# Three blocks of 512 tokens instead of four of 384 in a fused attention, dense and two-expert kernel

## The chip, the cores and the metric

The kernel runs on one core of a Trainium2 chip. The metric is device time in microseconds of the whole program, from one launch. A core has TensorE (PE; PEld is its weight load), VectorE (DVE), ScalarE (ACT), GpSimd (POOL), SyncE (SP) and 16 DMA engines, which run side by side and meet at semaphores.

## The reference, cut to what matters

```python
# attention: 2 batches, 8 heads, 768 positions, head size 64; a window of 128 keys and 4 sinks
x = attention(q, k, v)                        # becomes 1536 tokens x 512
h = x @ w_in                                  # dense layer, 512 -> 2048
x = (h - tanh(h)) @ w_out                     # 2048 -> 512
noisy = x @ w_gate + log1p(exp(x @ w_noise)) * noise      # 8 experts
top2 = indices of the two largest of noisy;  w = softmax over these two
for e in range(8):                            # 512 -> 1024 -> 512
    out[chosen e] += w * (relu(x @ w1[e]) @ w2[e])
```

All of it is float32. The kernel splits each operand of a large product into a rounded part (hi) and the rest (lo) and multiplies three times: hi by hi, lo by hi, hi by lo.

## The kernel before

The order of the instructions on each engine is written out by hand; engines wait on semaphores that count up. There are three stages.

1. Attention, pair of heads by pair of heads. Its output goes through two PSUM banks into `xT_hi` and `xT_lo` (transposed tokens), 384 positions at a time.
2. The dense layer, block by block of `BLK` = 384 tokens (`KB` = 3 tiles of 128, `NBLK` = 4 blocks). For each of 16 chunks `fc` of the hidden axis, TensorE runs `hidden(blk, fc)` (12 matmuls, 4 chunks of the model axis by 3 products, into bank 0 or 1), ScalarE and VectorE make h - tanh(h) in place and split it (`block_hidden`), and two chunks later TensorE runs `project` (3 matmuls for each of the `KB` tiles, summed over `fc` in banks 2 to 4). Block 0 is written out; blocks 1 to 3 are a hardware loop. In the next block's first chunks lies the routing of the one before: `gate_turn`, `gate_route` and `gate_end` turn the block's output rows (`turn_tokens`, 4 transposes a tile) and multiply them by the gate weights (`route`, 4 products a tile, 8 records in the trace), then VectorE chooses two experts (`route_noise`, `route_choose`), `rank_tokens` counts, `route_place` gives each token a row, and GpSimd's `scatter` sends each tile's rows to `sorted_x` in two indirect DMAs, one for each choice.
3. The experts, as 31 tiles of 128 sorted tokens, in order of expert. A tile has `up` (24 matmuls) and `down` (24). Between them its hidden rows go to memory and back (`hid_out`, `hid_in`, both on ScalarE's queue), so that VectorE can transpose them in 32x32 blocks. Weights come in a ring of two experts; SyncE asks for an expert's four pieces in two halves each (L610), GpSimd splits each piece (L672, L674). The splits and the scatters share GpSimd's queue.

Around the change the order is this. Behind the last block TensorE runs `turn_rows(0)`, the routing steps without cover, `up(0)`, `rank_tokens`, `turn_rows(1)`, `turn_hidden(0)`, `up(1)`, `down(0)`, and `down(1)`, in which `turn_rows(2)` sits: that one needs rows which are loaded only behind the very last scatter (SyncE L594 to L595). SyncE then waits until the ring slot of the first expert is free and asks for the third expert's weights (L598 to L612).

At the end GpSimd gathers each token's two results from `sorted_y` (`gather`, 12 tiles twice, L750), scales and adds the first six tiles (`combine`, L762 and L765), while VectorE adds the last six (L1424), and SyncE writes them out. Before the gathers of a block GpSimd waits for a number of stored tiles (`stores_i`), worked out for that block:

```python
            for blk in range(NBLK):
                stores = pool.value_load(stores_i[0:1, blk, kk:kk + 1], min_val=16, max_val=16 * TILES)
                pool.wait_ge(scattered, 16 * TOP * TT)
                pool.wait_ge(ys_stored, stores)
                for i in range(blk * KB, blk * KB + KB):
                    gather(kk, rows, i)
                    if kk == 0 and i >= 2:
                        scale(i - 2)
                    if kk == 1 and 2 <= i < TT - LATE + 2:
                        combine(i - 2)
```

Of the kernel before, what the change touches and what calls it, by code (L numbers as in the profile page):

```python
# [39 lines left out]
def build(nc, q, k, v, w_in, w_out, w_gate, w_noise, noise, w1, w2, out, n_sink, window):  # L40
# [11 lines left out]
    TT = TOK // P  # L52
    BLK = S // 2
    KB = BLK // P
# [6 lines left out]
    HALF = FC // 2  # L61
    CAP = TOK
    QUAD = 4
    LANE = P // QUAD
    LATE = 2 * KB
    SCALE = float(D) ** -0.5
# [5 lines left out]
    W0 = n_sink  # L72
    assert 2 * D == P and H // 2 == CH and QT == 6 and KB == 3 and n_sink <= SK and window <= P

# [3 lines left out]
    with ExitStack() as ctx:  # L78
# [41 lines left out]


        X_HI = take(PAIRS * S)
        X_LO = take(PAIRS * S)
        xT_hi = place_at("xT_hi", X_HI, [2 * PAIRS, BLK], F32R)
        xT_lo = place_at("xT_lo", X_LO, [2 * PAIRS, BLK], F32R)
        gathered_a = place_at("gathered_a", X_HI, [TT, DM])
        y_rows_all = place_at("y_rows", X_LO, [KB, DM])
        y_rows = [y_rows_all[:, kk, :] for kk in range(KB)]
        assert KB * DM == CH * BLK

# [67 lines left out]
        rank_t = bank[7][:, P:P + KB * E].rearrange("p (i e) -> p i e", e=E)  # L198
        r_ln_t = bank[5][:, 0:KB * E].rearrange("p (i e) -> p i e", e=E)
        r_is_zero_t = route_table(E)  # L200
# [47 lines left out]
        part([2 * G * BLK])  # L248
        x2T = [part([DM]) for u in range(2)]

# [86 lines left out]

        ys = place_at("ys", X_LO + KB * DM, [DM])
        behind_rows = X_LO + (KB + 1) * DM
        xs = place_at("xs", behind_rows, [DM])  # L340
        hid = place_at("hid", behind_rows + DM, [FE])
        xsT_at = behind_rows + DM + FE
        xsT_hi = [place_at(f"xsT_hi{b}", xsT_at + 2 * b * DM, [DM], F32R) for b in range(2)]
        xsT_lo = [place_at(f"xsT_lo{b}", xsT_at + (2 * b + 1) * DM, [DM], F32R) for b in range(2)]
        assert xsT_at + 4 * DM <= X_LO + PAIRS * S

# [7 lines left out]
        part([FE])  # L354
        hidT_lo.append(place_at("hidT_lo_last", xsT_at + 2 * DM, [FE], F32R))
        assert FE == 2 * DM
# [136 lines left out]
        def _(sp):  # L493
# [295 lines left out]
        def _(act):  # L789
# [25 lines left out]
            def attn_out(p, half):  # L815
                act.wait_ge(attn_ready, 2 * p + half + 1)
                act.copy(xT_hi[:, half * PAIRS + p, :], attn_bank[half][:, 0:BLK]).then_inc(attn_act, 1)

# [206 lines left out]
        def _(dve):  # L1025
# [29 lines left out]
            def attn_out(p, half):  # L1055
                dve.wait_ge(attn_act, 2 * p + half + 1)
                at = half * PAIRS + p
                dve.tensor_tensor(xT_lo[:, at, :], attn_bank[half][:, 0:BLK], xT_hi[:, at, :].bitcast(F32),
                                  ALU.subtract).then_inc(attn_dve, 1)

# [43 lines left out]
            def block_rows(blk, scattered_blocks=None):  # L1104
                dve.wait_ge(y_ready, blk * KB + 2)
                if scattered_blocks is not None:
                    dve.wait_ge(scattered, 16 * TOP * KB * scattered_blocks)
                dve.tensor_copy(y_rows[1], bank[3][:, :]).then_inc(x2_dve, 1)

            def block_turned(blk, kk):  # L1110
                dve.wait_ge(x2_turned, blk * KB + kk + 1)
                dve.tensor_copy(x2T[0][:, :], bank[5][:, :]).then_inc(x2T_dve, 1)

# [86 lines left out]
            block_rows(0)  # L1200
            dve.wait_ge(route_loaded, 96)
            dve.wait_ge(consts_ready, 13)

            dve.sem_inc(ranks_read, 1)
            with dve.Fori(1, NBLK) as blk:

                for fc in range(FC):
                    block_hidden(blk, fc)
                    if fc < 2:
                        block_turned(blk - 1, 2 * fc)  # L1210
# [218 lines left out]
        def _(pe):  # L1429
# [73 lines left out]
            def hidden(blk, fc):  # L1503
# [68 lines left out]
            def turn_tokens(kk):  # L1572
                for c in range(CH):
                    last = pe.transpose(bank[5 + kk % 2][:, c * P:(c + 1) * P],  # L1574
                                        y_rows_all[:, kk, c * P:(c + 1) * P], ident[:, :])
                last.then_inc(x2_turned, 1)

            def route(kk):
                for c in range(CH):
                    last = pe.matmul(bank[7][:, kk * 2 * E:(kk + 1) * 2 * E],  # L1580
                                     x2T[kk % 2][:, c * P:(c + 1) * P], w_route[:, c, :],
                                     start=c == 0, stop=c == CH - 1)
# [36 lines left out]
            pe.wait_ge(attn_dve, 2 * PAIRS)  # L1619
            pe.wait_ge(route_loaded, 96)  # L1620
            with pe.Fori(1, NBLK) as blk:
                for fc in range(FC):
                    hidden(blk, fc)

                    if fc < 3:
                        (gate_turn, gate_route, gate_end)[fc](blk - 1)
                    if fc == 7:
# [71 lines left out]
            turn_rows(0)  # L1699
            for step in (gate_turn, gate_route, gate_end):  # L1700
                step(NBLK - 1)
# [59 lines left out]
```

## Time and profile before

| what | value |
|---|---|
| median of 3 runs | 734.25 us (729.37 to 735.9) |
| the profiled execution, its own time | 733.36 us |
| its span, first to last instruction | 731.4 us |
| TensorE busy | 717.3 us, 98% |
| GpSimd busy | 445.5 us, 61% |
| VectorE busy | 372.2 us, 51% |
| ScalarE busy | 225.8 us, 31% |
| mean granted clock of TensorE | 0.997 |

The profiled execution took 1.96 us more than its span; that is what lies around the instructions. Times of the trace count from the span's start. The end of a matmul is modelled, so the pace of matmuls is read from the starts of two of them, not from the duration of one.

### The profile page before, as it was taken

The page shows a single profiled execution, that of the slowest core. Times are in us where ns is not written, and L with a number is a line of the kernel's source. Part 1 is how long each engine was busy: PE and PEld are TensorE (multiplying, and loading weights), DVE is VectorE, ACT ScalarE, POOL GpSimd, SP SyncE. Part 2 cuts the span into 40 slices and gives each one's busy share as a digit, 9 for nine tenths or more (in the row PEclk, how much of TensorE's full clock was granted, in tenths as well). Part 3 has the DMA queues.
Part 4 walks back from the last instruction along what each step waited for, and adds up shares of the span by engine and source line. Part 5 has one row for each costly group of instructions (what it writes and reads, how often), then busy time and mean ns, then how long its engine had stood idle before and what let it go on. Part 6 is the DMA issues. An engine that isn't in the chain of part 4 may idle for free.

```text
span 731.4 us, 12987 instructions
## 1 busy us (share of the span) xinstructions
PE 717.3 (98%) x3792; PEld 608.7 (83%) x3793; DVE 372.2 (51%) x908; ACT 225.8 (31%) x530; POOL 445.5 (61%) x252
## 2 busy tenths in 40 slices
PE   7999999999999999999999989999999999999997
PEld 6677899999989999999987868888888888888886
DVE  4777532233523442344246556565656555665644
ACT  6999622223222422332222122121121121221212
POOL 6988998000300030003976996959995999986774
PEclk9999999999999999999999999999999999999999
DMA  8743385000100020004373478869785978758776
GB/s 273 283 147 97 111 302 229 0 1 1 73 14 1 0 86 0 0 0 156 117 297 120 125 225 284 262 210 302 244 271 178 323 240 293 269 169 265 224 234 218
DMA packets 69838, 121.46 MB, mean 166 GB/s; under 512 B 8240, under 2 KB 35504, under 8 KB 69296
## 3 DMA queue, kind: packets, MB, share of 16 engines
q1 hardware_dynamic: 28000, 63.92, 25.9%
q10 hardware_dynamic: 37968, 44.58, 17.8%
q0 software_dynamic: 3840, 12.59, 5.4%
q8 instruction: 16, 0.26, 0.2%
q14 instruction: 14, 0.11, 0.0%
HBM read 81.74 MB, written 39.32 MB: 166 GB/s over the span
## 4 chain that ended last, share of the span: by engine, by line
PE 90%; DMA 5%; SPq 2%; DVE 1%; POOL 1%; issue 1%; ACT 0%; ACTq 0%; POOLq 0%; DVEq 0%
PE bank L1689 20%; PE bank L1657 20%; PE bank L1514 18%; PE bank L1564 18%; PE bank L1467 4%; PE bank L1458 3%; PE bank L1440 2%; DMA hid_lanes<-hid_by_lane 2%; PE bank L1580 2%; DMA hid_by_lane<-hid 1%; SPq L524 1%; DMA arena<-in_k 1%; PE bank L1574 1%; POOL sorted_x L720 1%; DMA xs<-sorted_x 1%
## 5 line engine op out<-in xcount | busy, mean ns | idle before, releaser
L720 POOL DMA_INDIRECT sorted_x<-y_rows,arena x24 | 23.5, 980 | 210.7 <-DVEq L1178 204.6
L674 POOL TENSOR_TENSOR ring<-ring_raw,ring 128x2048 fp32r<-128x2048 f32 x32 | 147.6, 4613 | 2.5
L1689 PE MATMUL bank<-ring,hidT_hi 128*128 (+1 forms) x448 | 138.5, 390 | 3.7 <-DVE hidT_lo L1262 3.7
L1657 PE MATMUL bank<-ring,xsT_hi 128*128 (+1 forms) x496 | 134.0, 392 | 0.4 <-DVE xsT_lo L1225 0.4
L672 POOL TENSOR_TENSOR ring<-ring_raw,ones 128x2048 fp32r<-128x2048 f32 x32 | 115.3, 3602 | 27.0 <-DMA ring_raw<-in_moe_w 26.9
L1564 PE MATMUL bank<-w_out_sb,gated_hi 128*128 128x512 f32 x384 | 119.8, 393 | 0.0
L1657 PEld LDWEIGHTS bank<-ring,xsT_hi 128*128 128x128 f32 x496 | 93.4, 189 | 20.1 <-issue 0.8
L1689 PEld LDWEIGHTS bank<-ring,hidT_hi 128*128 128x128 f32 x448 | 83.8, 188 | 21.9 <-issue 4.7
L1097 DVE TENSOR_TENSOR bank<-bank,arena 128x384 f32<-128x384 f32 x64 | 36.2, 566 | 123.4 <-ACT arena L857 121.7
L1689 PE MATMUL bank<-ring,hidT_lo 128*128 (+1 forms) x224 | 87.2, 389 | 0.0
L1514 PE MATMUL bank<-xT_hi,w_in_hi 128*128 (+1 forms) x256 | 86.9, 340 | 0.0
L1514 PE MATMUL bank<-xT_hi,w_in_lo 128*128 (+1 forms) x256 | 86.3, 337 | 0.0
L1514 PE MATMUL bank<-xT_lo,w_in_hi 128*128 (+1 forms) x256 | 85.9, 336 | 0.0
L1564 PEld LDWEIGHTS bank<-w_out_sb,gated_hi 128*128 128x128 f32 x384 | 70.9, 188 | 12.2
L1657 PE MATMUL bank<-ring,xsT_lo 128*128 (+1 forms) x248 | 76.8, 391 | 0.0
L1564 PE MATMUL bank<-w_out_sb,gated_lo 128*128 128x512 f32 x192 | 75.8, 395 | 0.0
L857 ACT ACTIVATE arena<-bank 128x384 f32<-128x384 f32 x64 | 31.5, 492 | 140.9 <-PE bank L1514 133.2
L951 ACT CAST hidT_hi<-bank 128x512 fp32r<-128x512 f32 x56 | 30.4, 590 | 132.4 <-PE bank L1689 85.8
L1241 DVE STREAM_TRANSPOSE bank<-hid_lanes 128x512 f32<-128x512 f32 x56 | 62.0, 1153 | 18.3 <-DMA hid_lanes<-hid_by_lane 18.2
L1657 PEld LDWEIGHTS bank<-ring,xsT_lo 128*128 128x128 f32 x248 | 46.8, 189 | 9.9
L1101 DVE TENSOR_TENSOR gated_lo<-bank,gated_hi 128x384 fp32r<-128x384 f32 x64 | 35.7, 558 | 37.8 <-ACT gated_hi L862 37.8
L943 ACT ACTIVATE hid<-bank 128x512 f32<-128x512 f32 x31 | 18.6, 599 | 112.8 <-PE bank L1657 107.9
(205 smaller groups left out, 1060.9 us busy)
## 6 DMA issues: line engine op xcount, KB each, us to landing
ring_raw<-in_moe_w SPq DMA_DIRECT2D x48, 512.0 KB, 5.5
hid_by_lane<-hid ACTq DMA_DIRECT2D x28, 512.0 KB
hid_lanes<-hid_by_lane ACTq DMA_DIRECT2D x28, 512.0 KB
ring_raw<-in_moe_w SPq DMA_DIRECT2D x8, 1024.0 KB, 6.5
sorted_y<-ys ACTq DMA_DIRECT2D x31, 256.0 KB
xs<-sorted_x ACTq DMA_DIRECT2D x100, 64.0 KB
sorted_y<-zeros SPq DMA_DIRECT2D x1, 4864.0 KB, 25.7
arena<-in_k SPq DMA_DIRECT2D x8, 520.0 KB, 4.5
```

Source lines behind the costliest of these rows:

```text
L672: pool.tensor_tensor(hi, raw, one_like(raw), ALU.mult).then_inc(rounded, 1)
L674: ins = pool.tensor_tensor(lo, raw, hi.bitcast(F32), ALU.subtract)
L720: pool.indirect_dma_start(out=sorted_x[:, :], out_offset=bass.IndirectOffsetOnAxis(ap=row_at[k][:, kk:kk + 1], axis=0), in_=y_rows_all[:, ...
L857: act.activation(tanh_h[fc % 2][:, :], bank[fc % 2][:, 0:BLK], ACT.Tanh).then_inc(tanh_ready, 1)
L951: act.copy(hidT_hi[b][:, half * BANK:(half + 1) * BANK], bank[3 + half][:, :]).then_inc(hidT_rounded, 1)
L1097: dve.tensor_tensor(bank[fc % 2][:, 0:BLK], bank[fc % 2][:, 0:BLK], tanh_h[fc % 2][:, :], ALU.subtract).then_inc(gated_ready, 1)
L1101: dve.tensor_tensor(gated_lo[fc % G][:, :], bank[fc % 2][:, 0:BLK], gated_hi[fc % G][:, :].bitcast(F32), ALU.subtract).then_inc(gated_spli ...
L1241: dve.transpose(bank[3 + half][:, :].rearrange("p (c i g) -> p g c i", c=EC // 2, g=QUAD), lane_blocks[:, :, half * (EC // 2):(half + 1) * ...
L1514: last = pe.matmul(bank[fc % 2][:, 0:BLK], w[:, at:at + P], x[:, bass.ds(blk * CH + c, 1), :].rearrange("p a s -> p (a s)"), start=c == 0 ...
L1564: last = pe.matmul(bank[2 + kk][:, :], g[fc % G][:, kk * P:(kk + 1) * P], w_out_sb[:, fc, w, :], start=fc == 0 and n == 0, stop=fc == FC - ...
L1657: last = pe.matmul(bank[banks + half][:, :], x[:, c * P:(c + 1) * P], ring[:, bass.ds(at * 2 * WE + (w + c * FE + half * BANK), BANK)], st ...
L1689: last = pe.matmul(bank[into][:, :], x[:, c * P:(c + 1) * P], ring[:, bass.ds(at * 2 * WE + (w + CH * FE + c * DM), DM)], start=c == 0 and ...
```

## The change

`BLK` becomes 512, so `KB` = 4 and `NBLK` = 3. The attention's output still comes in halves of 384 positions and is written into token order (`attended`), so that a block is any 512 columns of `xT`. `project` now sums into banks 2 to 5; the transposes of the routing go into those same banks once their rows are copied out, and all four tiles are turned in one step (`gate_turn`) and multiplied by the gate weights in the next (`gate_route`). The blocks run in plain token order. In SyncE's queue a wait for the fourth tile's read-back (`hid_read` of 32, the second `hid_in`) is put ahead of the third expert's weights.

```diff
-    BLK = S // 2
+    HALF_S = S // 2
+    BLK = BANK
...
-    LATE = 2 * KB
+    LATE = TT // 2
...
-        xT_hi = place_at("xT_hi", X_HI, [2 * PAIRS, BLK], F32R)
-        xT_lo = place_at("xT_lo", X_LO, [2 * PAIRS, BLK], F32R)
+        xT_hi = place_at("xT_hi", X_HI, [CH, TOK], F32R)
+        xT_lo = place_at("xT_lo", X_LO, [CH, TOK], F32R)
...
-        r_ln_t = bank[5][:, 0:KB * E].rearrange("p (i e) -> p i e", e=E)
+        r_ln_t = bank[7][:, 3 * P:3 * P + KB * E].rearrange("p (i e) -> p i e", e=E)
...
-            blk, kk = divmod(i, KB)
-            return (blk % B) * S + (blk // B) * BLK + kk * P
+            return i * P
+
+        def attended(x, p, half):
+
+            at = (p // CH) * S + half * HALF_S
+            return x[:, p % CH, at:at + HALF_S]
...
             sp.wait_ge(tables_ready, 1)
+
+            sp.wait_ge(hid_read, 32)
             ahead, landed = [first_loaded[3]] * 2, 32
             for e in range(RING, E):
...
-                act.wait_ge(x2_turned, blk * KB + 2)
-                act.copy(x2T[1][:, :], bank[6][:, :]).then_inc(x2T_act, 1)
+                for kk in (1, 3):
+                    act.wait_ge(x2_turned, blk * KB + kk + 1)
+                    act.copy(x2T[:, kk, :], bank[2 + kk][:, :]).then_inc(x2T_act, 1)
...
-                dve.wait_ge(y_ready, blk * KB + 2)
-                if scattered_blocks is not None:
-                    dve.wait_ge(scattered, 16 * TOP * KB * scattered_blocks)
-                dve.tensor_copy(y_rows[1], bank[3][:, :]).then_inc(x2_dve, 1)
+                for kk in (1, 3):
+                    dve.wait_ge(y_ready, blk * KB + kk + 1)
+                    if scattered_blocks is not None:
+                        dve.wait_ge(scattered, 16 * TOP * KB * scattered_blocks)
+                    dve.tensor_copy(y_rows[kk], bank[2 + kk][:, :]).then_inc(x2_dve, 1)
...
-                                         x[:, bass.ds(blk * CH + c, 1), :].rearrange("p a s -> p (a s)"),
+                                         x[:, c, bass.ds(blk * BLK, BLK)],
...
             def gate_turn(blk):
-
-                pe.wait_ge(x2_act, 2 * blk + 1)
+                for kk in range(KB):
+                    pe.wait_ge((x2_act, x2_dve)[kk % 2], 2 * blk + kk // 2 + 1)
+                    turn_tokens(kk)
+
+            def gate_route(blk):
 
                 pe.wait_ge(ranks_read, blk + 1)
-                turn_tokens(0)
-                pe.wait_ge(x2_dve, blk + 1)
-                turn_tokens(1)
-
-            def gate_route(blk):
-                pe.wait_ge(x2T_dve, 2 * blk + 1)
-                route(0)
-                pe.wait_ge(x2_act, 2 * blk + 2)
-                turn_tokens(2)
-                pe.wait_ge(x2T_act, blk + 1)
-                route(1)
-
-            def gate_end(blk):
-                pe.wait_ge(x2T_dve, 2 * blk + 2)
-                route(2).then_inc(logits_ready, 1)
+                for kk in range(KB):
+                    pe.wait_ge((x2T_dve, x2T_act)[kk % 2], 2 * blk + kk // 2 + 1)
+                    last = route(kk)
+                last.then_inc(logits_ready, 1)
```

## Rows read from the trace of the kernel before

**Rows 1.** The page, busy time (share of the span) xinstructions of each engine.

```profile
PE 717.3 (98%) x3792; PEld 608.7 (83%) x3793; DVE 372.2 (51%) x908; ACT 225.8 (31%) x530; POOL 445.5 (61%) x252
```

**Rows 2.** By stage: length, PE PEld DVE ACT POOL busy, clock, DMA, GB/s.

```profile
150.30:221.80 71.50, 71.50 (x378) 65.02 (x377) 27.07 (x87) 20.37 (x40) 6.03 (x6) 1.00 0.06 23
...
443.00:720.00 277.00, 276.37 (x1223) 228.63 (x1222) 164.16 (x202) 55.06 (x102) 230.89 (x92) 1.00 0.76 249
```

**Rows 3.** What TensorE waited for: us in total, times, longest.

```profile
PE bank L1689 <- DVE hidT_lo L1262: 3.7, 3, 1.9
...
PE bank L1639 <- DMA xs<-sorted_x: 0.4, 1, 0.4
```

**Rows 4.** Chain that ended last: start us, us, what, xinstructions.

```profile
144.03 2.10 PE bank L1514 x12
148.22 2.10 PE bank L1514 x12
...
376.23 6.87 PE bank L1657 x24
...
459.41 5.44 PE bank L1689 x24
```

**Rows 5.** The chain of waits, window of 360 to 446 us.

```profile
393.40 0.97 POOL sorted_x L720
...
394.68 2.72 DMA sorted_x<-y_rows,arena
...
398.17 4.11 DMA xs<-sorted_x
...
418.01 8.64 DMA hid_by_lane<-hid
...
426.67 7.15 DMA hid_lanes<-hid_by_lane
```

**Rows 6.** SyncE's issues of the third expert's first pieces.

```profile
417.38 9.06 SPq L610 DMA_DIRECT2D ring_raw<-in_moe_w  x4
```

**Rows 7.** ScalarE's DMA issues, 411 to 416 us.

```profile
411.94 0.41 ACTq L929 DMA_DIRECT2D hid_by_lane<-hid  x1
...
415.60 1.27 ACTq L937 DMA_DIRECT2D hid_lanes<-hid_by_lane  x1
```

**Rows 8.** Timeline of TensorE, 362 to 446 us [idle before <-releaser].

```profile
370.66 0.63 PE L1639 MATMUL bank<-ident,xs 128*128 128x128 f32 x4
...
424.24 0.72 PE L1689 MATMUL bank<-ring,hidT_hi 128*128 x2 [1.14 <-DVE hidT_lo L1262]
...
437.34 0.73 PE L1689 MATMUL bank<-ring,hidT_hi 128*128 x2 [1.95 <-DVE hidT_lo L1262]
```

**Rows 9.** GpSimd's timeline, last half of that expert's w1 split.

```profile
440.53 4.63 POOL L674 TENSOR_TENSOR ring<-ring_raw,ring 128x2048 fp32r<-128x2048 f32 x1
```

**Rows 10.** Granted clock (third number from the end) at up(0).

```profile
376.00:377.00 1.00, 1.00 (x4) 0.88 (x4) 0.16 (x2) 0.68 (x3) 1.00 (x1) 0.50 1.06 442
```

**Rows 11.** Timeline of TensorE in the loop, between two rounds of hidden.

```profile
161.47 1.06 PE L1580 MATMUL bank<-w_route,arena 128*128 128x16 f32 x8
...
163.67 0.42 PE L1514 MATMUL bank<-xT_hi,w_in_hi 128*128 x1
```

**Rows 12.** GpSimd's timeline in the tail [idle before <-releaser].

```profile
697.68 0.99 POOL L750 DMA_INDIRECT gathered_b<-sorted_y,arena  x1 [5.14 <-DMA sorted_y<-ys]
...
701.26 0.99 POOL L750 DMA_INDIRECT gathered_b<-sorted_y,arena  x1
...
709.97 0.99 POOL L750 DMA_INDIRECT gathered_b<-sorted_y,arena  x1 [1.72 <-DMA sorted_y<-ys]
...
720.93 0.95 POOL L750 DMA_INDIRECT gathered_b<-sorted_y,arena  x1 [0.30 <-issue]
```

**Rows 13.** The tile gathered_b: ns min/median/max, and landings.

```profile
L1424 DVE SCALAR_TENSOR_TENSOR gathered_a<-gathered_b,arena,gathered_a x6: 743/747/747, 721.8 to 725.1; 128x512 f32<-128x512 f32 x6
...
DMA to landing us min/median/max: 3.3/3.9/7.1
```

More of the change, by code:

```diff
@@ L62, in build @@
     CAP = TOK
+    ROUTE_LOADS = 16 * (2 + NBLK)
     QUAD = 4
     LANE = P // QUAD
-    LATE = 2 * KB
+    LATE = TT // 2
     SCALE = float(D) ** -0.5
@@ L72, in build @@
     W0 = n_sink
-    assert 2 * D == P and H // 2 == CH and QT == 6 and KB == 3 and n_sink <= SK and window <= P
+    assert 2 * D == P and H // 2 == CH and QT == 6 and KB == CH and TOK % BLK == 0 and n_sink <= SK and window <= P
     assert -(-TOP * (TOK - BLK) // E) >= 2 * P
@@ L118, in build @@
         noise_sb = sb("noise_sb", [P, TT, E])
+        column[0] = -(-column[0] // 32) * 32
         X_HI = take(PAIRS * S)
         X_LO = take(PAIRS * S)
-        xT_hi = place_at("xT_hi", X_HI, [2 * PAIRS, BLK], F32R)
-        xT_lo = place_at("xT_lo", X_LO, [2 * PAIRS, BLK], F32R)
+        xT_hi = place_at("xT_hi", X_HI, [CH, TOK], F32R)
+        xT_lo = place_at("xT_lo", X_LO, [CH, TOK], F32R)
         gathered_a = place_at("gathered_a", X_HI, [TT, DM])
-        y_rows_all = place_at("y_rows", X_LO, [KB, DM])
+        y_rows_all = place_at("y_rows", X_LO, [KB, TOK])[:, :, 0:DM]
         y_rows = [y_rows_all[:, kk, :] for kk in range(KB)]
-        assert KB * DM == CH * BLK
+        x2T = place_at("x2T", X_HI, [KB, TOK])[:, :, 0:DM]
+        assert DM == BLK
         RING_AT = take(RING * 2 * WE)
@@ L248, in build @@
         part([2 * G * BLK])
-        x2T = [part([DM]) for u in range(2)]
         used[0] = behind_routing
@@ L336, in build @@
         hidT_lo = [place_at("hidT_lo", hidT_at + FE, [FE], F32R)]
[L338 to L345, printed above, removed]
+        free = [X_LO + c * TOK + BLK for c in range(CH)]
+        xs = place_at("xs", free[0], [DM])
+        ys = place_at("ys", free[0] + DM, [DM])
+        hid = place_at("hid", free[1], [FE])
+        xsT_hi = [place_at(f"xsT_hi{b}", free[2 + b], [DM], F32R) for b in range(2)]
+        xsT_lo = [place_at(f"xsT_lo{b}", free[2 + b] + DM, [DM], F32R) for b in range(2)]
+        assert TOK - BLK >= 2 * DM
         hid_lanes = place_at("hid_lanes", ARENA + used[0], [FE])
@@ L354, in build @@
         part([FE])
-        hidT_lo.append(place_at("hidT_lo_last", xsT_at + 2 * DM, [FE], F32R))
+        hidT_lo.append(place_at("hidT_lo_last", free[3], [FE], F32R))
         assert FE == 2 * DM
@@ L816, in attn_out @@
                 act.wait_ge(attn_ready, 2 * p + half + 1)
-                act.copy(xT_hi[:, half * PAIRS + p, :], attn_bank[half][:, 0:BLK]).then_inc(attn_act, 1)
+                act.copy(attended(xT_hi, p, half), attn_bank[half][:, 0:HALF_S]).then_inc(attn_act, 1)
             act.wait_ge(pool_step, 2)
@@ L1056, in attn_out @@
                 dve.wait_ge(attn_act, 2 * p + half + 1)
-                at = half * PAIRS + p
-                dve.tensor_tensor(xT_lo[:, at, :], attn_bank[half][:, 0:BLK], xT_hi[:, at, :].bitcast(F32),
-                                  ALU.subtract).then_inc(attn_dve, 1)
+                dve.tensor_tensor(attended(xT_lo, p, half), attn_bank[half][:, 0:HALF_S],
+                                  attended(xT_hi, p, half).bitcast(F32), ALU.subtract).then_inc(attn_dve, 1)
             for p in range(PAIRS):
@@ L1104, in block_rows @@
             def block_rows(blk, scattered_blocks=None):
-                dve.wait_ge(y_ready, blk * KB + 2)
-                if scattered_blocks is not None:
-                    dve.wait_ge(scattered, 16 * TOP * KB * scattered_blocks)
-                dve.tensor_copy(y_rows[1], bank[3][:, :]).then_inc(x2_dve, 1)
+                for kk in (1, 3):
[3 more added lines that the diff above has]
+                    dve.tensor_copy(y_rows[kk], bank[2 + kk][:, :]).then_inc(x2_dve, 1)
             def block_turned(blk, kk):
                 dve.wait_ge(x2_turned, blk * KB + kk + 1)
-                dve.tensor_copy(x2T[0][:, :], bank[5][:, :]).then_inc(x2T_dve, 1)
+                dve.tensor_copy(x2T[:, kk, :], bank[2 + kk][:, :]).then_inc(x2T_dve, 1)
             steps = [0]
@@ L1200, in _ @@
             block_rows(0)
-            dve.wait_ge(route_loaded, 96)
+            dve.wait_ge(route_loaded, ROUTE_LOADS)
             dve.wait_ge(consts_ready, 13)
@@ L1208, in _ @@
                     block_hidden(blk, fc)
-                    if fc < 2:
-                        block_turned(blk - 1, 2 * fc)
+                    if fc == 0:
+                        block_turned(blk - 1, 0)
+                        block_turned(blk - 1, 2)
                     if fc == 3:
@@ L1573, in turn_tokens @@
                 for c in range(CH):
-                    last = pe.transpose(bank[5 + kk % 2][:, c * P:(c + 1) * P],
+                    last = pe.transpose(bank[2 + kk][:, c * P:(c + 1) * P],
                                         y_rows_all[:, kk, c * P:(c + 1) * P], ident[:, :])
@@ L1580, in route @@
                     last = pe.matmul(bank[7][:, kk * 2 * E:(kk + 1) * 2 * E],
-                                     x2T[kk % 2][:, c * P:(c + 1) * P], w_route[:, c, :],
+                                     x2T[:, kk, c * P:(c + 1) * P], w_route[:, c, :],
                                      start=c == 0, stop=c == CH - 1)
@@ L1619, in _ @@
             pe.wait_ge(attn_dve, 2 * PAIRS)
-            pe.wait_ge(route_loaded, 96)
+            pe.wait_ge(route_loaded, ROUTE_LOADS)
             with pe.Fori(1, NBLK) as blk:
@@ L1623, in _ @@
                     hidden(blk, fc)
-                    if fc < 3:
-                        (gate_turn, gate_route, gate_end)[fc](blk - 1)
+                    if fc < 2:
+                        (gate_turn, gate_route)[fc](blk - 1)
                     if fc == 7:
@@ L1699, in _ @@
             turn_rows(0)
-            for step in (gate_turn, gate_route, gate_end):
+            for step in (gate_turn, gate_route):
                 step(NBLK - 1)
```

## The prediction

> **What bounds the kernel now.** I read the page first: TensorE is busy 98% of the span, its own weight load, which overlaps, 83%, and the next engine, GpSimd, 61% [rows 1]. The windows by stage say it is the same in each large stage: a block of the dense layer's loop has no idle time on TensorE in 71.5 us, and the steady part of the experts 0.6 us in 277 [rows 2]. So the kernel is as long as TensorE's list of instructions, plus the few places where it waits. TensorE's waits name them: 3.7 us for the transposed hidden rows, in three waits, and 0.4 us for the rows of tile 2 [rows 3]; all of those lie where one stage hands over to the next or at the very end. A change in block size can then do four things: alter the pace of matmuls, alter the work between blocks, and shift the two hand-overs, where queues on GpSimd and the DMAs end last.
>
> **The change part by part.** The sums are against the profiled execution, 733.36 us (span 731.4), which is 0.9 us under the median of the runs.
>
> Matmuls of `hidden`. Before: 4 blocks x 16 x 12 = 768 of 384 columns; after 3 x 16 x 12 = 576 of 512, the same columns. In the chain a group of 12 takes 2.10 us, 175 ns each, 134.4 us in all [rows 4]. No row has this product at 512 columns. The nearest are the experts' matmuls, 24 in 5.44 us, or 226.7 ns, and `project` beside today's `hidden`: from one `hidden` to the next are 4.19 us, less 2.10 leaves 2.09 for 9, or 232 ns [rows 4]. Times 576 that is 130.6 or 133.6 us, a gain of 3.8 or 0.8. I take 229 ns, between them, for `hidden` will have an eviction beside it as `project` has but is otherwise the experts' form: 131.9 us, **-2.5** (-3.8 to -0.8). `project` has 576 matmuls of 512 before and after: nothing.
>
> The Trainium skill ("TensorE: Matmul & The Clock Gate", section "Wait — 56ns, not 53.3ns?") has start-to-start at the full clock as the columns over 2.4 GHz and a fixed 2.5 ns. By that page 192 matmuls fewer would save 0.5 us, and the total below would be 2.0 us more. The trace does not agree: 175 ns at 384 columns and 227 at 512 are 13 to 15 ns above the columns' time [rows 4].
>
> Evictions of `hidden` grow by a third each, and there are a quarter fewer. VectorE is busy 27.07 us and ScalarE 20.37 of a block's 71.5 [rows 2], the bank is wanted again only two projections and one `hidden` later (6 us now, 8 after), and the four steps on one chunk are a fraction of that. Hidden by TensorE's own matmuls, cost 0; without the cover it would be their whole growth, some 0.7 us a chunk.
>
> Work between blocks. It goes by tiles, and there are 12 before and after. What is saved is one of the loop's three rounds of `rank_tokens` and its seams, and the short wait of `route` behind the last block for a copy (four turns in a row now give that copy time). I take **-0.8** (-1.2 to 0).
>
> The last scatter. The last block's tokens are placed by VectorE, then sent by GpSimd, one indirect DMA every 1.28 us (393.40 to 394.68) [rows 5]. Eight instead of six are 2.6 us more, and the placing has one more step in its chain and slightly wider ones, 0.2 us. Behind it nothing has slack: landing 2.72 us, then SyncE's load of 4.11 us, and TensorE is already waiting 0.4 us for it [rows 3, 5]. Queued behind that wait are the rest of `down(1)` and `up(2)`, so all of it counts: **+2.8** (2.5 to 3.6). GpSimd's splits of the second expert come 2.6 us later too; TensorE comes 2.8 later as well, so they stay as hidden as they are.
>
> The third expert's weights. SyncE asks for them at 417.38, when `up(3)` has freed the slot [rows 6]. From 418.01 the write of tile 3's hidden rows takes 8.64 us and its read 7.15, while tile 2's write, issued at 411.94, had landed when the read behind it went out at 415.60, 3.7 us later [rows 5, 7]. The weights are the large stream that starts between the two. With them held back until that read has landed, both steps should take near 3.7 us: the read is issued about 423 and lands by 427 to 428 instead of 433.8. TensorE waits for it 1.95 us at 437.3, and 1.14 us for tile 2's read at 424.2 [rows 8]. Both go: **-3.0** (-3.1 to 0). What is queued behind the new wait is all of SyncE's weight loads. Piece 0 would be asked for near 428 and land near 435; GpSimd is free for it about 429, so it starts some 6 us later than now. Now the w1 half is split at 445.2 [rows 9], and would be near 451; `up(8)`, the first to use it, starts at 464.9 (the chain's step at 459.41 and 5.44 more) [rows 4]. The w2 half must wait for `down(3)` in either kernel. Cost 0, as long as less than 13 us are lost; past that each is a microsecond on TensorE.
>
> The clock. Behind the last block TensorE ran transposes and `route` (16 columns wide) from 370.66 until 376.2, and the granted clock then stood at 0.50, the 1.2 GHz level; `up(0)` took 6.87 us for what 5.44 pays elsewhere, a loss of 1.4 [rows 4, 8, 10]. In the loop such work stands in shorter pieces, the longest 2.2 us (161.47 to 163.67, two routes and one turned tile), at a clock of 1.00 throughout [rows 2, 11]. After the change `gate_route` is four routes in a row, about 3.5 us, twice in the loop; behind the last block the thin work grows from 5.5 to about 6 us; and the longer wait for the scatter is an idle gap of 3.2 us. Each of the three new stretches is longer than those that kept the clock and shorter than the one that lost it, and no row shows which they resemble. I take one more loss: **+1.4** (0 to +4.3, three of 1.43).
>
> The tail. Which tiles a block's gathers need follows from the reference's routing of its inputs: the last expert has tiles 25 to 28 (counting from 0), and of its 393 tokens, 95, 204, 303 and 393 have come by the end of the four old blocks, 131, 264 and 393 by that of the new. So the second-choice gathers wait for 26, 27, 28 and 29 stored tiles before, and for 27, 28 and 29 after. The trace shows the middle two: GpSimd resumes at 697.68 and 709.97, each behind a store [rows 12]. Before, tiles 0 to 2 were gathered ahead of the first wait, so by 709.97 six gathers were out; after, only four (0 to 3). A gather with a `combine` takes 3.57 us (697.68 to 701.26), a bare one 1.27. From the second resumption the new order is 4 x 3.57 + 3 x 1.27 = 18.1 us until the last gather starts, at 728.1 (before: 720.93). It lands 3.3 to 3.9 us later, its combine takes 0.75, and the write of those 256 KB about 2 to 2.7, an estimate from the scatter of as much, which landed in 2.72 [rows 5, 12, 13]. That is 734.1 to 735.5, against the 731.4 at which TensorE's last store now ends the span. If the store ahead of the second wait lands 1.6 us earlier, since fewer gathers run beside it, the end is 1.6 earlier too. I take **+2.5** (1.2 to 4.0): the end passes from TensorE's chain to GpSimd's.
>
> Sum: -2.5 -0.8 +2.8 -3.0 +1.4 +2.5 = **+0.4**, 733.36 + 0.4 = 733.8 us.
>
> **The rivals.**
> (a) The covers hold better: no further loss of clock, the tail at its low end, the matmuls at 226.7 ns. -3.8 -0.8 +2.8 -3.0 +0 +1.2 = -3.6, **729.8 us**. For it: the experts' matmuls have exactly this form. Against: `project` shows 232 in the very place.
> (b) Slower: GpSimd's queue is the bound at both hand-overs, with eight scatters in a row and four gathers behind each store wait. In the tail it decides from the point where the second store wait ends later than 706.5 (731.4 less 18.1, 3.6, 0.75 and 2.4); beyond that each microsecond counts, and so it does from the first at the scatter. With 3.6 and 4.0 for the two and the rest as forecast that is +2.3 over it, and with `hidden` at 232 ns another 1.7: **737.8 us**. For it: the scatter wait has no slack, the store wait ended at 709.97. Against: DMAs that the change itself thins out.
> (c) The moved request does not do what it says: the 8.64 us write is slow through its own packets or other transfers, and both waits of TensorE stay. +3.0 over the forecast: **736.8 us**. For it: the write and the read are both of 512 KB in small packets; against: 3.7 us one tile earlier.
> (d) The clock falls in both loop rounds and behind the scatter wait: +2.9 over the forecast, **736.7 us**. The Trainium skill has the idle one of these in "TensorE: Matmul & The Clock Gate", section "Why this matters for your kernels": idle gaps between bursts of matmuls bring the lower clock back. By the trace the gap of 1.95 us did not, for the stretch behind it runs at 1.00; the 5.5 us of thin work did [rows 2, 8, 10].
>
> **How the numbers follow.** Forecast 0.42, (a) 0.20, (b) 0.13, (c) 0.11, (d) 0.14. About 1% (7.3 us) is what a measurement of this kernel can tell from no change: its three runs lie 6.5 us apart. All five cases are inside that. All bounds at their low end make 729.0 us, at their high end 744.5. Over 740.7 two or three of the costs of (b), (c) and (d) must meet, which I give 0.08; a gain over 7.3 us is more than all bounds allow and would be an error of mine in the list itself, 0.05. The range of 8 in 10 leaves out most of the stacked cases and takes in the spread of the runs at its low side: 728 to 739.
>
> **What would show it.** Starts of `hidden` matmuls 226 to 232 ns apart; eight scatters behind the last block and a TensorE wait of about 3 us for `xs`; a write of tile 3's hidden rows near 4 us and no wait for `hidT_lo` there; the granted clock in the loop behind `gate_route`; the chain of waits ending in `gathered_b`, VectorE and the output write. The prediction is wrong if the 512-column matmuls leave that band, if the weights of the third expert reach TensorE late, or if a loop block shows idle time on TensorE.

## The result, and the profile after

The changed kernel takes 743.2 us (median of 4 runs, 741.29 to 745.25) against 732.46 for the kernel before (median of 4, 729.37 to 735.9): ratio 1.0146, 95% interval 1.0088 to 1.0204. The forecast was 733.8, with a range to 739: wrong, and on the slower side. The profiled execution of after took 745.25 us (span 743.5), 2 us over its median; that of before is the one of the prediction (733.36, span 731.4). So the two spans differ by 12.2 us, the medians by 10.7.

The page of after (header, busy time as in [rows 1], and the granted clock in 40 slices):

```profile
span 743.5 us, 12373 instructions
PE 726.9 (98%) x3596; PEld 588.1 (79%) x3597; DVE 368.7 (50%) x836; ACT 217.3 (29%) x493; POOL 446.3 (60%) x252
PEclk8999999999999999999998999999999999999998
```

TensorE has 196 instructions fewer and is busy 9.6 us longer. Idle time grew too, but most of the loss is inside the work. Where, is told by cutting the span at the first matmul of a few places, in either trace:

| stretch, from the first matmul of one to the next | before | after | after less before |
|---|---|---|---|
| start to `hidden` | 83.91 | 84.43 | +0.5 |
| dense layer, to `turn_rows(0)` | 286.75 | 286.66 | -0.1 |
| to `up(0)` | 5.41 | 5.71 | +0.3 |
| to `up(6)` | 66.86 | 68.93 | +2.1 |
| to `up(29)` | 250.24 | 254.53 | +4.3 |
| to the last matmul | 34.28 | 33.98 | -0.3 |
| to the end of the span | 3.9 | 9.3 | +5.4 |

The chain that ended last, of after (start us, us, what, xinstructions):

```profile
186.23 3.48 PE bank L1590 x32
189.71 4.45 PE bank L1524 x12
...
285.87 4.37 PE bank L1524 x12
...
376.95 7.17 PE bank L1659 x24
...
451.36 5.60 PE bank L1691 x24
456.96 5.47 PE bank L1659 x24
...
735.16 4.80 DMA gathered_b<-sorted_y,arena
```

L1590 is `route`, L1524 `hidden`, L1574 `project`, L1641 `turn_rows`, L1659 `up`, L1691 `down`. Three things are to be seen. The `hidden` behind `route` takes 4.4 us, in both rounds of the loop, where its neighbours take 2.76 (below, under the third experiment). A `down` takes 5.60 us; in [rows 4] it is 5.44, and nothing of `down` was changed. And the chain ends on GpSimd's gathers, where before it ended on TensorE's last store.

The windows around the first `route` of the loop and around TensorE's wait for the rows of tile 2 (as in [rows 2]: length, busy times, granted clock, DMA):

```profile
184.00:188.00 4.00, 4.00 (x29) 3.62 (x27) 2.35 (x4) 1.68 (x4) 0.00 (x0) 1.00 0.01 4
188.00:192.00 4.00, 4.00 (x23) 3.46 (x23) 0.69 (x1) 0.21 (x1) 0.00 (x0) 0.75 0.01 2
...
403.00:407.00 4.00, 1.15 (x5) 1.15 (x6) 0.00 (x0) 0.00 (x0) 3.92 (x2) 0.75 0.28 103
407.00:411.00 4.00, 4.00 (x10) 3.09 (x10) 3.06 (x16) 0.59 (x1) 4.00 (x2) 0.50 0.21 66
```

TensorE was busy all the time from 184 to 192, and yet the clock fell from 1.00 to its lower level, 1.2 GHz, for part of the second window. At 403 it had been idle, waiting for the rows of tile 2; there the fall slowed four transposes and 21 matmuls behind it. TensorE's wait there, and the chain around it:

```profile
PE bank L1641 <- DMA xs<-sorted_x: 3.5, 1, 3.5
```

```profile
398.50 3.83 DMA sorted_x<-y_rows,arena
...
403.10 2.70 DMA xs<-sorted_x
405.85 1.13 PE bank L1641 x4
406.98 3.84 PE bank L1691 x9
410.82 3.30 PE bank L1659 x12
```

The wait is 3.5 us where it was 0.4 [rows 3], +3.1. What the fall adds is read from the starts: from the first transpose to the end of these 12 of `up` are 8.11 us, and 5.45 in experiment 2 below, which had the wait and no fall, so 2.7. In return the hidden rows of tile 3 come in time. ScalarE's queue (issues of the write and of the read):

```profile
424.12 0.40 ACTq L938 DMA_DIRECT2D hid_by_lane<-hid  x1
427.70 0.34 ACTq L946 DMA_DIRECT2D hid_lanes<-hid_by_lane  x1
```

The write that took 8.64 us [rows 5] has landed after 3.6, and TensorE no longer waits there for `hidT_lo` [rows 3, 8]: -3.1. One more wait is gone that [rows 3] does not show. In the kernel before it is, for tile 1:

```profile
PE bank L1689 <- DVE hidT_lo_last L1262: 0.7, 1, 0.7
```

### The profile page after: what moved, and what is told of

Read it like the earlier page. It is cut to its first block, busy times and chain, and to the rows that moved or that the text cites. A ratio compares the mean times of both kernels' runs of the same rounds, so it can differ in the third digit from the quotient of the medians.

```text
span 743.5 us, 12373 instructions
## 1 busy us (share of the span) xinstructions
PE 726.9 (98%) x3596; PEld 588.1 (79%) x3597; DVE 368.7 (50%) x836; ACT 217.3 (29%) x493; POOL 446.3 (60%) x252
## 4 chain that ended last, share of the span: by engine, by line
PE 90%; POOL 4%; DMA 3%; issue 1%; DVE 1%; ACT 1%; SPq 0%; POOLq 0%; DVEq 0%
PE bank L1659 22%; PE bank L1691 19%; PE bank L1524 18%; PE bank L1574 18%; PE bank L1477 4%; PE bank L1468 3%; PE bank L1450 3%; PE bank L1590 1%; POOL gathered_b L758 1%; POOL sorted_x L728 1%; DMA arena<-in_k 1%; PE bank L1584 1%; DMA gathered_b<-sorted_y,arena 1%; POOL gathered_b L770 1%; POOL gathered_a L773 1%
## 5 line engine op out<-in xcount | busy, mean ns | idle before, releaser
L1691 PE MATMUL bank<-ring,hidT_hi 128*128 (+1 forms) x448 | 141.1, 396 | 0.0
L1659 PE MATMUL bank<-ring,xsT_hi 128*128 (+1 forms) x496 | 135.0, 394 | 0.4 <-DVE xsT_lo L1235 0.4
L1574 PE MATMUL bank<-w_out_sb,gated_hi 128*128 128x512 f32 x384 | 120.9, 396 | 0.0
L1659 PEld LDWEIGHTS bank<-ring,xsT_hi 128*128 128x128 f32 x496 | 94.1, 190 | 20.9 <-issue 0.6
L1105 DVE TENSOR_TENSOR bank<-bank,arena 128x512 f32<-128x512 f32 x48 | 33.6, 699 | 137.5 <-ACT arena L865 137.5
L1691 PEld LDWEIGHTS bank<-ring,hidT_hi 128*128 128x128 f32 x448 | 84.0, 188 | 19.6
L1691 PE MATMUL bank<-ring,hidT_lo 128*128 (+1 forms) x224 | 88.6, 395 | 0.0
L1574 PEld LDWEIGHTS bank<-w_out_sb,gated_hi 128*128 128x128 f32 x384 | 72.2, 188 | 16.5
L1524 PE MATMUL bank<-xT_hi,w_in_hi 128*128 (+1 forms) x192 | 77.5, 404 | 0.0
L1659 PE MATMUL bank<-ring,xsT_lo 128*128 (+1 forms) x248 | 77.4, 394 | 0.0
L1524 PE MATMUL bank<-xT_hi,w_in_lo 128*128 (+1 forms) x192 | 76.6, 399 | 0.0
L1524 PE MATMUL bank<-xT_lo,w_in_hi 128*128 (+1 forms) x192 | 75.9, 395 | 0.0
L1574 PE MATMUL bank<-w_out_sb,gated_lo 128*128 128x512 f32 x192 | 75.7, 394 | 0.0
L865 ACT ACTIVATE arena<-bank 128x512 f32<-128x512 f32 x48 | 28.7, 598 | 155.3 <-PE bank L1524 151.8
L1251 DVE STREAM_TRANSPOSE bank<-hid_lanes 128x512 f32<-128x512 f32 x56 | 66.5, 1232 | 11.4 <-DMA hid_lanes<-hid_by_lane 11.4
L1659 PEld LDWEIGHTS bank<-ring,xsT_lo 128*128 128x128 f32 x248 | 47.0, 189 | 10.2
L1691 PEld LDWEIGHTS bank<-ring,hidT_lo 128*128 128x128 f32 x224 | 42.1, 188 | 10.2
```

The lines of the kernel that those rows point to most:

```text
L865: act.activation(tanh_h[fc % 2][:, :], bank[fc % 2][:, 0:BLK], ACT.Tanh).then_inc(tanh_ready, 1)
L1105: dve.tensor_tensor(bank[fc % 2][:, 0:BLK], bank[fc % 2][:, 0:BLK], tanh_h[fc % 2][:, :], ALU.subtract).then_inc(gated_ready, 1)
L1251: dve.transpose(bank[3 + half][:, :].rearrange("p (c i g) -> p g c i", c=EC // 2, g=QUAD), lane_blocks[:, :, half * (EC // 2):(half + 1) * ...
L1524: last = pe.matmul(bank[fc % 2][:, 0:BLK], w[:, at:at + P], x[:, c, bass.ds(blk * BLK, BLK)], start=c == 0 and n == 0, stop=c == CH - 1 an ...
L1574: last = pe.matmul(bank[2 + kk][:, :], g[fc % G][:, kk * P:(kk + 1) * P], w_out_sb[:, fc, w, :], start=fc == 0 and n == 0, stop=fc == FC - ...
L1659: last = pe.matmul(bank[banks + half][:, :], x[:, c * P:(c + 1) * P], ring[:, bass.ds(at * 2 * WE + (w + c * FE + half * BANK), BANK)], st ...
```

## Experiments

Eleven runs of ten kernels; experiment 6 ran one of them twice. The kernel before was run beside them each time; its medians were 729.0 to 729.9 us, some 3 us under the 732.46 of the result. The changed kernel itself was not run again, so its 743.2 stands against the 732.46 alone.

**1. Where the experts' time went.** `down` and its operands are the same in both kernels, but not their places. The tables of the routing grew with `KB`, and `hidT_at` follows behind them without alignment. Between the start of `hidT` (stationary) and that of the weight ring (moving) lie, modulo 256 bytes, 0 bytes before and 64 after. In the kernel before I shifted `hidT` by 16 columns, to the same 64 bytes. The two tiles behind it in the arena, `hid_lanes` and `hidT_hi_last` (tile 1's `hidT_hi`), move with it; nothing else does:

```diff
+        used[0] += 16
         hidT_at = ARENA + used[0]
```

> The kernel before, with every tile from hidT on moved by 16 columns (64 bytes in each partition) and nothing else. In the changed kernel the 24 matmuls of a down take 5.60 us instead of 5.44, and there the transposed hidden rows happen to start 64 bytes off a 128-byte boundary. Theory P (place): the place of hidT is the cause. Then a down takes 5.60 us here too and the span grows by 27 x 0.15 = 4 us, to about 735.5. Rival S (state): the slower pace comes from something else in the changed kernel (its DMAs, its instruction stream), and the place is chance. Then 5.44 and no change, 731.4.

Measured 735.56 us against 729.69, ratio 1.0084 (1.0058 to 1.011). Its chain:

```profile
500.76 5.60 PE bank L1690 x24
506.36 5.47 PE bank L1658 x24
511.83 5.60 PE bank L1690 x24
```

`down` slows to 5.60 and `up` to 5.47, to the digit of after; the stretch from `up(6)` to `up(29)` takes 254.5 us. The whole +4.3 us of after is reproduced by a shift of 64 bytes. Over all 31 tiles, at 0.19 us each, it makes 5.8 us, and the medians differ by 5.9.

**2. Which boundary.** In the changed kernel the same 16 columns make the difference 128 bytes:

> The changed kernel with hidT 16 columns further, which puts it on a 128-byte boundary again. Theory P with a boundary of 128 bytes: a down takes 5.44 us again, and the span is 4.3 us shorter than 743.5. Rival Q: what counts is that the stationary and the moving operand start alike modulo 256 bytes; here hidT is 128 bytes off the ring by that measure, so a down stays near 5.55 to 5.60. Rival S: 5.60 unchanged.

One run: 740.33 us. `down` is as slow as at 64 bytes:

```profile
501.89 5.59 PE bank L1692 x24
507.47 5.46 PE bank L1660 x24
```

The addresses settle two rivals. `hidT` and `hid_lanes` start at 128 modulo 256 bytes here, as they do in the kernel before; only the ring stands elsewhere (0 instead of 128). So it is neither the place of `hidT` alone nor that of `hid_lanes`, but the difference of the two operands.

**3. A difference of 0, for `hidT` and for `gated` too.** `gated` (stationary of `project`) and `w_out` (moving) start alike before and 128 bytes apart after:

```diff
+        used[0] += 32
         gated_at = ...
...
+        used[0] += 48
         hidT_at = ARENA + used[0]
```

> The changed kernel with hidT 48 columns further (like the ring modulo 256 bytes) and the gated tiles of the dense layer 32 columns further (like w_out modulo 256 bytes). Theory P and rival Q both expect a down of 5.44 us, 4.3 us less. Rival Q alone expects project to get faster too: now its 36 matmuls behind a block take 8.37 us, 232.5 ns each, against 227 to 228 in the kernel before; with like starts 36 would take 8.2 us, and the 576 of project and the first of each hidden together some 2 to 3 us less. Theory P leaves project at 232.5.

Measured 732.87 us against 729.69, ratio 1.0045 (1.0023 to 1.0067). The same two kinds of group, first in this kernel, then a group of `project` in it (L1576) and in after (L1574), with the `hidden` ahead of it:

```profile
506.08 5.44 PE bank L1661 x24
511.52 5.44 PE bank L1693 x24
```

```profile
358.71 2.72 PE bank L1526 x12
361.43 8.16 PE bank L1576 x36
```

```profile
360.12 2.76 PE bank L1524 x12
362.88 8.37 PE bank L1574 x36
```

In these groups `down`, `up` and `project` are at 226.7 ns per matmul; about two thirds of what the change cost is gone (ratio 1.0146 to 1.0045). `hidden`, whose own operands start alike in every kernel here, also goes from 2.76 to 2.72 for 12.

**4. Four routes in a row, or two and two.** In the loop the last two routes go behind the next `hidden`, as a `gate_end`:

```diff
             def gate_route(blk):
                 pe.wait_ge(ranks_read, blk + 1)
-                for kk in range(KB):
+                for kk in range(2):
                     ...
                     route(kk)
+            def gate_end(blk):
+                for kk in range(2, KB):
...
-                    if fc < 2:
-                        (gate_turn, gate_route)[fc](blk - 1)
+                    if fc < 3:
+                        (gate_turn, gate_route, gate_end)[fc](blk - 1)
```

> The changed kernel with two of the four routes one chunk later (behind hidden 2 of the next block), so that the piece of thin work in the loop is 1.75 us instead of 3.5. In the changed kernel the granted clock fell to 0.50 behind both of the loop's gate_route, and the hidden that follows took 4.4 us instead of 2.8. Theory C: the length of the thin piece is the cause; then no fall in the loop and 3.3 us less than 743.5. Rival: it is all thin work of the block together, turns included, wherever it stands; then the falls stay and so does the time.

One run: 739.5 us. The window of the loop (after has 0.98 there), and the dense layer takes 283.41 us instead of 286.66, which is the predicted -3.3 against before:

```profile
150.00:360.00 210.00, 210.00 (x964) 172.96 (x963) 70.32 (x192) 52.70 (x89) 40.34 (x22) 1.00 0.10 37
```

Over all profiled executions, the clock fell in or right behind 9 of 12 stretches of four routes in the loop, behind none of 6 with the routes split, and behind none of 12 in the order of before. The 16 transposes of `gate_turn` stand in a row in all of these changed kernels, with one `hidden` between them and the routes; only the routes were split.

**5. The moved wait taken back**, in the changed kernel (`sp.wait_ge(hid_read, 32)` removed):

> The changed kernel without the wait for the fourth tile's read-back ahead of the third expert's weights. Theory W: the weights slow the write and the read of tile 3's hidden rows, so TensorE's waits for hidT_lo of 1.1 and 1.9 us come back, +3.0 us. Rival: the changed order around the last scatter (its longer wait) had already spread these transfers, and the wait does nothing: same time, no waits of TensorE for hidT_lo.

One run: 742.48 us. The chain of waits:

```profile
419.70 7.28 DMA hid_by_lane<-hid
427.00 6.55 DMA hid_lanes<-hid_by_lane
```

The slow write is back, so it is the weights' stream that slows it. But TensorE's waits behind it are 0.8 us for tile 3 and 0.2 for tile 2, where before they were 1.95 and 1.14 [rows 8], and from `turn_rows(2)` to `up(6)` this kernel takes 40.15 us against 38.76 in experiment 8, which has the moved wait and a fall of the clock of the same length behind the same wait. So it is worth 1.4 us here, not 3.0. Part of the reason lies in the row itself: the kernel before does not always wait 3.1 us. In experiment 1, with the request where it was, the same waits are:

```profile
PE bank L1690 <- DVE hidT_lo L1263: 1.4, 2, 0.9
```

**6. The moved wait alone, in the kernel before**, run twice:

```diff
             sp.wait_ge(tables_ready, 1)
+            sp.wait_ge(hid_read, 32)
```

> The kernel before with this wait alone. Theory W: the write of tile 3's rows takes near 4 us instead of 8.6, TensorE's two waits there go, -3.0 us, span 728.4. Rival: the transfers are slow through their own packets, or the third expert comes late; then 731.4 or more.

Measured 727.19 us against 729.02, ratio 0.9981 (0.9959 to 1.0003); in the repetition 727.5 against 729.91, 0.9968 (0.9946 to 0.9991).

> The kernel before with the new wait alone, once more and in five rounds, for its size: in three rounds the ratio was 0.998 with an interval of 0.996 to 1.000. Theory W with the waits as in the first profile: 0.996. If other executions have shorter waits there (1.4 instead of 3.1 us, as in e1): 0.998.

Its waits of TensorE, as in [rows 3]:

```profile
PE bank L1690 <- DVE hidT_lo L1263: 0.4, 1, 0.4
```

One wait of 0.4 us stands where there were two of 1.95 and 1.14. The profiled execution is 5.0 us shorter from `up(0)` to `up(6)`, but 1.3 of that is a fall of the clock behind the last block that this execution did not have. By the medians the gain is 1.8 and 2.4 us. The first interval just takes in 1, the second does not: this half of the change is good by itself, if small.

**7. Work in the wait for the scatter.** 14 matmuls that nobody reads, put ahead of `turn_rows(2)` into the wait:

```diff
+                        for _ in range(14):
+                            pe.matmul(bank[1][:, :], hidT_hi[b][:, 0:P], ring[:, 0:BANK], start=True, stop=True)
```

> The changed kernel with 14 matmuls of 512 columns, whose result nobody reads, ahead of turn_rows(2), where TensorE waits 3.5 us for the last scatter. They take 14 x 0.227 = 3.2 us of that wait. Theory C: the idle gap makes the clock fall (0.50 from 404.8 to 411.6 us), which costs 3.0 us; with the gap filled the clock stays at 1.00 and the span is 3.0 us shorter although work was added. Rival: the fall has another cause (the transposes and the thin work around it), the matmuls run inside the gap and the time stays.

One run: 741.74 us, no fall there, and from `up(0)` to `up(6)` 65.22 us instead of 68.93; 1.6 of that is the fall behind the last block, which this execution did not have either. It proves little alone: experiments 2 and 3 had no fall there either, with the wait left idle. Over all profiled executions the clock fell in 5 of 7 idle waits of 2.4 to 3.6 us, and in neither of two that were filled.

**8. The tail.** `LATE` = 8 leaves four instead of six combines to GpSimd, so that its last gathers start sooner:

```diff
-    LATE = TT // 2
+    LATE = TT - 4
```

> The changed kernel with VectorE adding the last eight tiles instead of six, so that GpSimd has four combines instead of six. Theory G: the end of the program is GpSimd's list behind the second store wait; with two combines of 2.3 us fewer between gathers the last gather starts near 729.5 instead of 735.2, and the end passes back to TensorE's last store: about 738 instead of 743.5, -5.5 us. Rival: the gathers wait for their own landings or for the stores, and nothing or only 1 to 2 us is won.

Measured 740.25 us against 729.02, ratio 1.0167 (1.014 to 1.0195); in the profile 6.3 us from the last matmul to the end instead of 9.3. The chain of its end:

```profile
725.00 2.11 PE bank L1691 x9
...
727.13 0.59 ACT ys L966
...
727.75 5.25 DMA sorted_y<-ys
...
733.08 0.59 ACT ys L966
```

The last gather started at 727.18, 8 us sooner, and the end is TensorE's own again: the last copy into `ys` must wait until a store of the buffer's last contents has landed, and that store takes 5.25 us. So 3.0 us came of the 5.5 expected.

**9. Placement and split routes together** (the edits of 3 and 4):

> The changed kernel with both placements (hidT and the gated tiles like the ring and w_out modulo 256 bytes) and with the routes split over two chunks. If the causes found so far are independent, this is the larger block without its two costs in the dense stage: from the first hidden to the end of the last projection 281.5 us (286.8 before, 286.7 changed), a down of 5.44 us, and what is left over the kernel before are the longer scatter wait with its fall of the clock and the tail: a span of 731 to 733, a ratio to before of 1.000 to 1.004. Rival: the falls of the clock move to other places (behind the turns, or behind each half of the routes), and the dense stage stays above 284.

Measured 729.78 us against 729.91, ratio 0.9987 (0.9961 to 1.0013). The dense layer takes 278.68 us, 8.1 less than before. This is the forecast's case, no difference, with the gain larger than forecast and the tail (9.7 us) dearer.

**10. All four**, with 10 filling matmuls and `LATE` = 8 added to 9:

> The same with ten matmuls in the scatter wait and eight tiles summed by VectorE. Independent causes: 3 us less from the tail and 0 to 3 from the clock at the scatter wait, a span near 727, a ratio of 0.993 to 0.997 to the kernel before, level with the kernel before that has the new wait alone. Rival: the tail only moves to the last store, which shares the DMAs with the outputs, and gives 1 us.

Measured 726.25 us against 729.91, ratio 0.994 (0.9915 to 0.9964): this beats the kernel before and the changed one. But most of it is the moved wait: against the kernel before with that wait alone (experiment 6, 727.5 us, measured beside it) the ratio is 0.998, 1.3 us. Larger blocks with their losses mended bring little more. Its windows by stage:

```profile
20.00:360.00 340.00, 340.00 (x1914) 276.53 (x1911) 137.89 (x426) 128.57 (x309) 136.54 (x104) 1.00 0.24 86
360.00:371.00 11.00, 11.00 (x76) 10.12 (x75) 6.08 (x26) 4.53 (x9) 7.21 (x2) 1.00 0.71 271
371.00:431.00 60.00, 59.02 (x275) 48.44 (x274) 38.05 (x123) 12.90 (x22) 45.60 (x18) 1.00 0.54 190
431.00:700.00 269.00, 269.00 (x1188) 222.75 (x1187) 161.54 (x198) 53.62 (x99) 226.24 (x81) 1.00 0.76 248
```

No fall of the clock in any stage, and 1 us of idle time on TensorE from 20 to 700. What is left is the tail, 9.2 us, in spite of `LATE`:

```profile
712.09 7.49 DMA gathered_b<-sorted_y,arena
...
719.61 0.75 DVE gathered_a L1436
```

Against the last matmul the last gather goes out 3.5 us sooner than in 9, but lands 2.5 us later after its issue (7.49 against 5.04), and the write behind it takes 0.6 more: 0.5 us is left. Five other gathers were issued in the 7 us ahead of it; that they are what slows it was not tried.

## Why the prediction was wrong

The steps, against the two profiled spans and the experiments:

| step | forecast | measured | by |
|---|---|---|---|
| matmuls of `hidden` and work between blocks | -3.3 | -3.4, with the clock's falls taken out | table above, experiment 4 |
| `project` unchanged | 0 | in that sum; about 3 us too slow by its operands' places | 3, 9 |
| last scatter | +2.8 | +3.1 | wait for `xs` |
| third expert's weights | -3.0 | -3.1 in this pair; 1.4 and 1.8 to 2.4 by experiment | 5, 6 |
| clock | +1.4 | +6.3 | chain, starts |
| tail | +2.5 | +5.4 | chain |
| steady part of the experts | not in the list | +4.3 | 1 to 3 |
| start, hand-over to `up(0)`, last tiles | not in the list | +0.5 | table |

These sum to +13.1 where the spans differ by 12.2. Of the missing 0.9, 0.7 is tile 1's wait for `hidT_lo_last`, which is gone too; the rest I can't place. (The third wait of [rows 3] is also gone, but it lay in the last tiles, whose stretch is in the sum.) The forecast's sum was +0.4. The result also lies over 740.7, a case to which I gave 0.08.

**The step that failed is the list itself.** I wrote that the kernel is as long as TensorE's list of instructions, and costed only edited instructions. But "`project` has 576 matmuls of 512 before and after: nothing" and the untouched experts both rest on operands staying where they were against each other, and the diff moves them: more `KB` means longer tables ahead of `gated` and `hidT` and other starts for all that follows. The new places cost 4.3 us in the steady part of the experts, shown by experiment 1 in the old kernel and taken away by 3, and 4.7 in the dense layer (283.41 in experiment 4, 278.68 in 9, which differ in placement alone). The diff did show that buffers moved; I read them only for overlap.

**The dense term was right by two errors.** With starts alike, the dense layer gains 8.1 us, not 3.3. By mean distances of starts in the loop, `hidden` goes from 176.5 to 228.0 ns (experiment 9): 768 x 176.5 less 576 x 228.0 is 4.2 us, a little past its low bound. `project` goes from 232.0 to 228.0, 576 times, 2.3 us: blocks of 512 speed it up, where I took the 232 of [rows 4] as its nature. The rest, 1.6, is the work between blocks, for which I had allowed 0.8, and what I can't place. The change spoiled its own gain by placement, and the sum came out as forecast.

**The clock: rival (d)'s mechanism.** I took one more loss of 1.4 us; there were three (1.7, 1.6 and 2.7) and the known one grew by 0.3. I had [rows 11] as proof that thin work in the loop is harmless and did say that the new stretch is longer than any that kept the clock; the value 1 of 3 was a choice between ends without a row. Also a fall was priced at 1.4 us, from the one row; behind the wait for the scatter it cost 2.7, since it lasted longer and hit `turn_rows(2)` and 21 full matmuls. By the Trainium skill ("TensorE: Matmul & The Clock Gate", section "Why this matters for your kernels") idle gaps bring the lower clock back; the wait at 403 agrees, as do five of the seven such waits, while two (3.30 and 2.42 us, experiments 2 and 3) brought no fall. The two falls in the loop have no gap ahead of them (4.00 of 4.00 us busy from 184 to 188). The Trainium skill (the same page, section "Part 4: PE-mode transpose") says that transposes do not count as busy in the same way. In experiment 4 the transposes kept their place and number and the fall went with the splitting of the 16-column products alone, so the transposes by themselves did not bring it. Whether the products would without the transposes 2.8 us ahead of them, no run shows.

**The tail: rival (b)'s half.** The mechanism was forecast, the order of gathers and the engine that ends the span too. From the end of the second store wait I had 18.1 us to the last gather's start, 3.6 to its landing, 0.75 and 2.4, together 24.9. GpSimd's timeline of after:

```profile
715.40 0.99 POOL L758 DMA_INDIRECT gathered_b<-sorted_y,arena  x1 [1.68 <-DMA sorted_y<-ys]
...
735.16 1.34 POOL L758 DMA_INDIRECT gathered_b<-sorted_y,arena  x1 [1.69 <-DMA gathered_b<-sorted_y,arena]
```

That is 19.8, then 4.80, 0.75 and 2.8 for the write, together 28.1, +3.2. The 1.69 in brackets is the wait I left out: `gather` lets only so many be under way, and the last waits until the one three before has landed. The wait for the store ended 1.4 us sooner against TensorE's last matmul than before; I had taken 0.9 off for that (from +3.4 to +2.5). The landings of [rows 13] lie between 3.3 and 7.1. I took 3.6; the last gather of before landed in 3.98, that of after in 4.80.

**What was right.** The wait for the scatter (+3.1 against +2.8), the write of tile 3's hidden rows (3.6 us), no wait of TensorE for the third expert, no idle time in the loop, evictions without cost.

`hidden` too is 1% slower in after (230.2 against 228.0 ns from start to start), with its own operands alike. The starts tell where: by medians its first seven matmuls, behind a slow `project`, take 224 to 236 ns and its last 232, while the eighth to eleventh take 227, like all of them in experiment 9. In the experts the first six matmuls of an `up` behind a slow `down` are the slow ones in the same way. So a misplaced group also slows the start of the next group, which is why `up` goes from 5.44 to 5.47.

Not settled: why that is so; why `project` before paces 232 with starts alike (the nine behind a `hidden` of 384 columns take 224 to 236 ns each, and only in the row of 27 at a block's end do the later ones reach 227; no experiment here took that apart); and whether thin products alone make the clock fall. The clock's falls differ between executions of kernels with the same order (one or two in the loop, by execution), so a single run of 2, 4, 5 and 7 is read by its stretches, not by its total.

## What to carry to other kernels

When a size changes, list again every buffer's start behind it, and compare stationary and moving operands of each large matmul modulo 256 bytes: an untouched stage lost 1.7% by that here (254.53 against 250.24 us). Count the microseconds that TensorE spends in a row on narrow products and transposes, and keep them in pieces between full matmuls; an idle wait can be filled. Coarser blocks save seams but lengthen what is queued where a stage hands over, scatters at one end and gathers at the other, and there nothing covers it.

## What the runs showed of the hardware

In the experts a matmul of 512 columns with its weight load starts every 226.7 ns when both operands start alike modulo 256 bytes (24 in 5.44 us), and every 233 ns in `down` when they differ by 64 or by 128 (5.60 and 5.59 us). The absolute place did not matter: `down` takes 5.44 with both starts at 128 modulo 256 in the kernel before and with both at 0 in experiment 3. The Trainium skill ("SBUF — State Buffer", section "Operand start alignment") asks only for a multiple of the element's size; every kernel here obeys that, fast or slow.

The granted clock fell with TensorE busy without a gap (1.00 to 0.75 over 184 to 192), behind 3.5 us of 16-column products. Of the indirect gathers of 128 rows that were issued about 3.6 us apart, most landed in 3.3 to 3.6 us and a few later (4.29, 5.21 and, in the kernel before, 7.14). As the last of a burst it landed in 3.98 (before), 4.80 (after), 5.70, 5.04 and 7.49 us (experiments 8, 9 and 10); what sets this was not tried.
